# Moving the transposes of one more pair of heads from TensorE to VectorE and DMAs, and scoring one group a product earlier

## The reference

```
scores = cap * tanh(q @ k.T / sqrt(64) / cap)
attn   = exp(scores - max) / (sum + 1e-9);  x = attn @ v    # heads joined: (4*448, 768)
h = sigmoid(x @ w_gate) * (x @ w_val)                       # d_ff 1536   first product
z = h @ moe_w_out                                           # 768         second product
g = z @ moe2_w_in;  g = g * cos(g)                          # d_ff 2048   third product
y = g @ moe2_w_out                                          # 768         fourth product
```

## Time and profile before

| what | value |
|---|---|
| median of 3 runs | 1210.89 us (1210.07 to 1212.64) |
| the profiled execution, its own time | 1212.21 us |
| its span, first to last instruction | 1210.2 us |
| TensorE busy | 1199.9 us, 99% of the span |
| VectorE, ScalarE, GpSimd busy | 621.4, 508.4, 516.7 us |
| mean granted TensorE clock | 0.997 of full speed |
| moved by DMAs | 298.77 MB, mean 247 GB/s |

### The profile page before, as it was taken

The page is one execution under the profiler, slowest core; times in us unless marked ns, Lnnn a source line. Parts: engine busy times, 40 slices in busy tenths (PEclk is TensorE's granted clock), DMA queues, the critical chain, the costliest instruction groups (busy, mean ns, idle before and its releaser), DMA issues.

```text
span 1210.2 us, 16764 instructions
## 1 busy us (share of the span) xinstructions
PE 1199.9 (99%) x5932; PEld 1089.3 (90%) x5932; DVE 621.4 (51%) x1227; ACT 508.4 (42%) x957; POOL 516.7 (43%) x458
## 2 busy tenths in 40 slices
PE   8999999999999999999999999999999999999998
PEld 6779989999999999989999999999999999999998
DVE  8951148876773466766651265777662211105610
ACT  8941145656541445546640245545661011105610
POOL 7969968879753346662104406674302100000000
PEclk8999999999999999999999999999999999999999
DMA  5579987799776699999678769999768566666663
GB/s 162 161 243 317 316 308 235 241 319 321 291 284 238 224 262 259 255 262 285 235 238 272 254 194 271 263 275 258 262 227 283 191 221 216 212 221 220 239 233 108
DMA packets 150034, 298.77 MB, mean 247 GB/s; under 512 B 60480, under 2 KB 69440, under 8 KB 149952
## 3 DMA queue, kind: packets, MB, share of 16 engines
q1 hardware_dynamic: 134064, 287.37, 71.9%
q10 hardware_dynamic: 15888, 10.33, 3.2%
HBM read 219.39 MB, written 58.98 MB: 230 GB/s over the span
## 4 chain that ended last, share of the span: by engine, by line
PE 94%; ACT 2%; DVE 1%; DMA 1%; SPq 1%; issue 0%; ACTq 0%
PE acc L842 27%; PE acc L841 27%; PE acc L843 27%; PE s_ps L739 3%; PE s_ps L740 3%; PE acc L794 2%; PE t_ps L811 2%; PE t_ps L813 1%; PE t_ps L776 1%; PE acc L831 1%; PE t_ps L760 1%; PE acc L833 1%; SPq L484 1%; ACT h_lo_whole L1041 0%; DMA pt_lo_whole<-h_lo_whole 0%
## 5 line engine op out<-in xcount | busy, mean ns | idle before, releaser
L841 PE MATMUL acc<-h_hi,w_hi 128*128 128x448 f32 x672 | 247.4, 368 | 0.0
L842 PE MATMUL acc<-h_lo,w_hi 128*128 128x448 f32 x672 | 245.6, 366 | 0.0
L843 PE MATMUL acc<-h_hi,w_lo 128*128 128x448 f32 x672 | 245.5, 365 | 0.0
L841 PE MATMUL acc<-x_hi,w_hi 128*128 128x448 f32 x576 | 211.3, 367 | 0.0
L842 PE MATMUL acc<-x_lo,w_hi 128*128 128x448 f32 x576 | 211.0, 366 | 0.0
L843 PE MATMUL acc<-x_hi,w_lo 128*128 128x448 f32 x576 | 210.9, 366 | 0.0
L562 POOL TENSOR_TENSOR pt_lo<-pt_lo_whole,pt_hi 128x1344 fp32r<-128x1344 f32 x24 | 74.5, 3105 | 220.7 <-ACT pt_hi L1069 220.7
L843 PE MATMUL acc<-z_hi,w_lo 128*128 128x448 f32 x384 | 140.2, 365 | 0.0
L841 PE MATMUL acc<-z_hi,w_hi 128*128 128x448 f32 x384 | 140.2, 365 | 0.0
L842 PE MATMUL acc<-z_lo,w_hi 128*128 128x448 f32 x384 | 140.2, 365 | 0.0
L843 PEld LDWEIGHTS acc<-h_hi,w_lo 128*128 128x128 f32 x672 | 126.2, 188 | 10.1
(11 more groups left out here) (138 smaller groups left out, 1976.4 us busy)
## 6 DMA issues: line engine op xcount, KB each, us to landing
w_lo<-w_pair SPq DMA_DIRECT2D x156, 384.0 KB, 4.0
w_hi<-w_pair SPq DMA_DIRECT2D x156, 384.0 KB, 3.4
w_lo_whole<-w SPq DMA_DIRECT2D x52, 384.0 KB, 3.8
w_pair<-w_lo SPq DMA_DIRECT2D x52, 384.0 KB, 4.4
w_pair<-w_hi SPq DMA_DIRECT2D x52, 384.0 KB, 4.9
w_lo<-w_pair SPq DMA_DIRECT2D x36, 512.0 KB, 4.4
w_hi<-w_pair SPq DMA_DIRECT2D x36, 512.0 KB, 3.7
qk_in_whole<-qk SPq DMA_DIRECT2D x35, 512.0 KB, 5.9
```

Source lines behind the costliest of these rows:

```text
L841: e.matmul(out[:, 0:S], w_hi[u % HI][:, wb, :], a_hi[:, kb, :], start=first, stop=False)
L842: e.matmul(out[:, 0:S], w_hi[u % HI][:, wb, :], a_lo[:, kb, :], start=False, stop=False)
L843: return e.matmul(out[:, 0:S], w_lo[u % LO][:, wb, :], a_hi[:, kb, :], start=False, stop=last)
```

## The change

`MOVED` becomes 11: pair 11 is transposed by VectorE and moved by DMAs as well. Its blocks go to SP at the last three halves of batch 0 (`moves_of_first`), the last quarter of each head to ScalarE at steps 18 and 20. Its low parts are written by VectorE, by a `moved_low` there, not by POOL. Group 41 is scored within the third product, after its first half unit; so all later groups are scored, exponentiated and normalised one step earlier, and `prob` has two more tiles to hold them.

```diff
-MOVED = 2 * PAIRS
+MOVED = 2 * PAIRS - 1
+BETWEEN = NG * PAIRS + FOURTH_0 + AHEAD
-    prob = sb("prob", [P, TILES - 1, S])
+    prob = sb("prob", [P, TILES + 1, S])
     def scored_at(b, n):
+        if b == 0 and n >= FOURTH_0:
+            return group_of(b, n + AHEAD + 1) if FOURTH_0 < n < STEPS - AHEAD - 1 else None
+        return group_of(b, n + ahead(b)) if n + ahead(b) < STEPS else None
     def scored_before(b, n):
+        n += AHEAD if b == 0 and n >= FOURTH_0 else ahead(b) - 1
+        return group_of(b, n) if 0 <= n < STEPS else None
     def prob_of(g):
-        if g < NG * MOVED:
+        if g < NG * MOVED and g != BETWEEN + 1:
             return last_prob if ts[0] == TILES - 1 else prob[:, ts[0]:ts[-1] + 1, :]
-        at = moved_no(g) % 3 * 2
+        at = moved_no(g) % NG * 2 if g >= NG * MOVED else TILES - 1
...
 # SP, and the like in ScalarE's move_blocks
-                    e.wait_ge(s_pv, max(2 * (pr - 1) + d + 1, 2 * MOVED))
+                    e.wait_ge(s_pv, 2 * (pr - 1) + d + 1)
+                    if pr == MOVED:
+                        e.wait_ge(s_tr, TILES * MOVED)
+            def moves_of_first(n):
+                d, last = divmod(n - len(halves) + 3, 2)
+                if d >= 0:
+                    move_blocks(MOVED, d, (0, 1, 2) if d == 1 else (2,) if last else (0, 1))
...
                         if n >= KEEP_LATER:
                             keep(*halves[n - KEEP_LATER])
+                        moves_of_first(n)
...
 # TensorE
             def times_v(b, i, d):
-                    g = NG * i + 3 + d 
+                    g = NG * i + 3 + d + (NG * i >= FOURTH_0)
             def third_product(b):
                         m.then_inc(s_acc, 1)
+                        if b == 0 and j == 0 and h == 0:
+                            e.wait_ge(s_tanh, BETWEEN + 1)
+                            scores(BETWEEN + 1, s_ps)
...
 # ScalarE, attend
-                if b > 0 and n % 2 == 0 and 0 <= n + 2 < STEPS and n != FOURTH:
+                if n % 2 == 0 and 0 <= n + 2 < STEPS and pair_of(b, (n + 2) // NG) >= MOVED and (b == 0 or n != FOURTH):
                     move_last_blocks(b, n)
 # ScalarE, end of second_product
-                    tanh(group_of(b, FOURTH_0 + AHEAD))
+                    tanh(BETWEEN)
+                    tanh(BETWEEN + 1)
...
 # VectorE
+            def moved_low(pr, d):
+                e.wait_ge(s_pbhi, 2 * (pr - MOVED) + d + 1)
+                at = of_head(d)
+                e.tensor_tensor(pt_lo[:, 0:CH, at], pt_whole[:, 0:CH, at], f32(pt_hi)[:, 0:CH, at],
+                                ALU.subtract).then_inc(s_pblow, 1)
+                e.wait_ge(s_pblow, 2 * (pr - MOVED) + d + 1)
+                e.tensor_tensor(pt_hi[0:D, CH, at], pt_whole[D:P, CH, at], f32(pt_hi)[D:P, CH, at],
+                                ALU.subtract).then_inc(s_pb, 1)
             def attend(b, n):
+                i, r = divmod(n, NG)
+                if b == 0 and NG * MOVED <= group_of(b, n + AHEAD - 1) < group_of(b, STEPS):
+                    turn_blocks(group_of(b, n + AHEAD - 1))
+                if b == 0 and i < PAIRS and pair_of(b, i) >= MOVED and r in (1, 3):
+                    moved_low(pair_of(b, i), r // 2)
...
 # VectorE, end of second_product
-                    row_max(group_of(b, last + 1))
+                    row_max(BETWEEN)
+                    row_max(BETWEEN + 1)
```

More of the change, by code:

```diff
@@ L288, in scored_at @@
     def scored_at(b, n):
-        return group_of(b, n + ahead(b)) if n + ahead(b) < STEPS and (b > 0 or n != FOURTH_0) else None
+        if b == 0 and n >= FOURTH_0:
+            return group_of(b, n + AHEAD + 1) if FOURTH_0 < n < STEPS - AHEAD - 1 else None
+        return group_of(b, n + ahead(b)) if n + ahead(b) < STEPS else None
     def scored_before(b, n):
-        return group_of(b, n + ahead(b) - 1) if 0 <= n + ahead(b) - 1 < STEPS and (b > 0 or n != FOURTH_0) else None
+        n += AHEAD if b == 0 and n >= FOURTH_0 else ahead(b) - 1
+        return group_of(b, n) if 0 <= n < STEPS else None
     def step_of(b, stage, j, h):
@@ L328, in prob_of, with last_there @@
         ts = GROUPS[g % NG]
-        if g < NG * MOVED:
+        if g < NG * MOVED and g != BETWEEN + 1:
             return last_prob if ts[0] == TILES - 1 else prob[:, ts[0]:ts[-1] + 1, :]
-        at = moved_no(g) % 3 * 2
+        at = moved_no(g) % NG * 2 if g >= NG * MOVED else TILES - 1
         return prob[:, at:at + len(ts), :]
+    def last_there(g):
+        return {BETWEEN + 1: g - 2 * NG, BETWEEN + 1 + NG: g - 2 * NG, BETWEEN + 3 + NG: BETWEEN + 1}.get(g, g - NG)
     def turned_by_tensor(b, n):
@@ L920, in third_product @@
                             e.wait_ge(s_o, 2 * (pair_of(b, PAIRS // 2 - 1) - ALONE) + h + 1)
-                            e.wait_ge(*normalised(tiles_of(group_of(b, FOURTH_0 + AHEAD - 1))[-1]))
+                            e.wait_ge(*normalised(tiles_of(BETWEEN - 1)[-1]))
                         else:
@@ L986, in _ @@
                 if b == 0:
-                    between = group_of(b, FOURTH_0 + AHEAD)
-                    e.wait_ge(s_tanh, between)
-                    scores(between, s_ps)
+                    e.wait_ge(s_tanh, BETWEEN)
+                    scores(BETWEEN, s_ps)
                 third_product(b)
@@ L1014, in tanh @@
                 e.wait_ge(s_score, g + 1)
-                if moved_no(g) >= 3:
-                    e.wait_ge(s_blocks, moved_no(g) - 3 + 1)
+                if moved_no(g) >= NG:
+                    e.wait_ge(s_blocks, moved_no(g) - NG + 1)
                 elif g >= NG * (ALONE + 1):
-                    e.wait_ge(s_tr, tiles_of(g - NG)[-1] + 1)
+                    e.wait_ge(s_tr, tiles_of(last_there(g))[-1] + 1)
                 e.activation(prob_of(g), at[:, 0:len(ts), 0:S], ACT.Tanh,
@@ L1108, in attend @@
                         x_high(pr)
-                i, r = divmod(n + 1, NG)
-                if b > 0 and 0 <= i < PAIRS and r in (0, 2) and i != FOURTH // NG:
+                i, r = divmod(n + 1 if b > 0 else n, NG)
+                if 0 <= i < PAIRS and r in (0, 2) and pair_of(b, i) >= MOVED and i != first_of_fourth(b) // NG:
                     moved_high(pair_of(b, i), r // 2)
@@ L1150, in second_product @@
                 if b == 0:
-                    exp(group_of(b, FOURTH_0 + AHEAD - 1))
+                    exp(BETWEEN - 1)
                 z_high(b, U2 - 1)
@@ L1409, in second_product @@
                 if b == 0:
-                    last = FOURTH_0 + AHEAD - 1
-                    normalise(group_of(b, last), zeros[0])
-                    row_max(group_of(b, last + 1))
+                    normalise(BETWEEN - 1, zeros[0])
+                    row_max(BETWEEN)
+                    row_max(BETWEEN + 1)
             def third_product(b):
```

## The result

The changed kernel takes 1222.3 us (median of 6 runs, 1219.8 to 1225.4), the kernel before 1211.7 in the same comparison: a ratio of 1.0091 (95% interval 1.0071 to 1.0111), 10.6 us slower. The direction was forecast; the size was not: +3.2 was predicted, and 1222.3 lies above the range of 1209.2 to 1218.2. The profiled execution took 1222.1 us with a span of 1220.3, against 1210.2 before.

What follows compares the result with a forecast made beforehand. TensorE, busy 1199.9 of 1210.2 us, bounds the kernel. Late weights for batch 1's second half unit give +3.2, holding the 2.7 saved and step 13's wait: 1215.4 against the profiled run, 1214.1 against the median; range 1209.2 to 1218.2.

Steps and rivals of the forecast that it cites:

- What can be gained, 2.7 us: TensorE's stream loses 25 transposes of pair 11 at 0.11 us each: 2.7 us, 0.23% of the time.
- The rival of 6.8 us: Each of the 25 transposes costs its full 273 ns on TensorE, 6.8 us saved, total 1207.3; chance 0.02.
- Step 12, a wait of 1.9 us more: ScalarE's exponential ahead of the high parts makes TensorE's transposes at step 13 wait 1.9 us more (1.1 to 2.3).
- The blocks ready at 354.3, SP's queue waiting for them: SP's first moves of pair 11 wait for VectorE's turn of group 45 until 354.3, with loads and keeps behind.
- SP's chain: SP issues moves, loads and keeps from 354.3; last keeps start at 372.6, all kept at 382.6, 11.5 us later.
- My upper bound: SP and weights: 0.7 us an issue, VectorE 1.7 later, keeps 11 us, what follows 11.5: a loss of 8 us.
- Step 21, a wait of 0.3 us (0 to 3): TensorE waits 0.3 us for head 0's low part, ready at 371.5, hidden in the later wait for weights.
- The waits for weights, 0.7 and some 3 us: TensorE waits for DMAs at batch 1's first and second half units, 0.7 and some 3 us.
- a sign of being wrong: The prediction counts as wrong if TensorE waits at steps 21 and 23; size not given.
- the small pieces fill the DMA queues: Pair 11's moves in 448-byte pieces run at half rate, delaying blocks and keeps: +5 to +8, say 1217.5; chance 0.08.
- It cancels: SP, the keeps or VectorE are quicker, weights come between 388.5 and 392.6: within 2.4 us of before, say 1211; chance 0.32.
- the moves are hidden: All keeps pass before 377.5, no weights late, step 12 costs under 0.3 us: 2.4 to 2.7 gained, 1208.3; chance 0.11.

Runs made afterwards that it cites:

- Kernel ten: Kernel of eight, but batch 1's loads wait only for their own unit's and buffer's keeps, and group 40's normalisation reads other zeros: 1209.8 us, ratio 0.9985.
- experiment nine: Kernel of eight, but all three last keeps are issued behind head 1's moves, where two stood ahead: 1215.7 us, ratio 1.0032.
- experiment two: Changed kernel, but TensorE takes head 0's product with v one step later, at step 22: 1223.1 us, ratio 1.0091.
- seven: Changed kernel with last loads and two keeps no longer behind all pair 11 moves, and step 12's high parts before the exponential: 1216.3 us, ratio 1.0039.
- eight: Kernel of seven, but head 0's product with v comes a step later, at step 22: 1211.8 us, ratio 0.9998.
- experiment one: Changed kernel, but batch 1's loads wait only for their own unit's and buffer's keeps, last three keeps spread over three half units: 1219.4 us, ratio 1.0065.
- third kernel: Changed kernel with the edits of experiment one and experiment two together: 1218.3 us, ratio 1.0053.
- five: Changed kernel with SP's order altered: the last two loads and their keeps no longer stand behind all pair 11 moves: 1218.0 us, ratio 1.0051.
- the fourth: Only the earlier scoring of group 41 and later groups; TensorE transposes pair 11 as before: 1214.2 us, ratio 1.0023 against the kernel before.

## Why the prediction was right in its direction and wrong in its size

- *What can be gained, 2.7 us:* right as far as it can be seen. Kernel ten has the transposes gone and nearly no new wait, and its -1.8 (-0.4 to -3.3) agrees with 2.4. The rival of 6.8 us is outside.
- *Step 12, a wait of 1.9 us more:* right: 2.0 us of waits against 0.2, and for the reason given. The exponential now stands ahead of the high parts:

```profile
314.18 0.77 ACT L1045 ACTIVATE prob<-prob,shift,cap_abs 128x448 f32<-128x448 f32 x1
...
315.68 0.48 ACT L1083 ACTIVATE pt_hi<-t_ps 128x384 fp32r<-128x384 f32 x1
```

  The fall of the clock that can follow such a wait was not in the sum.
- *The blocks ready at 354.3, SP's queue waiting for them:* right, 355.1. The window of 350 to 355 us shows the cost of the idle queue, a DMA share of 0.00 in the changed kernel:

```profile
350.00:355.00 5.00, 5.00 (x28) 4.61 (x27) 4.87 (x12) 2.02 (x5) 2.97 (x2) 1.00 0.00 0
```

- *SP's chain, the term that failed:* I let 24 moves take 15.5 us at the 0.64 to 0.7 us of the earlier trace rows wherever they stood. They took 5.3 + 4.3 + 9.8 = 19.3, since sixteen of them followed weight DMAs that still filled the queues, as experiment nine shows. With small terms besides (0.8 at the start, 1.1 in the loads, keeps and gaps) the last keeps came at 378.3, not 372.6, and with 0.5 more in the drain the loads at 388.7, not 382.6: 6.1 us late of what was forecast. That is most of the 7.4 us by which the total was too low. The largest part is 3.8 us of issues, and the earlier trace rows already held the sign of it: behind 1.5 MB issued from 339.46 on, the load at 340.94 took 1.24 us to issue, where the one at 339.46 took 0.43. My upper bound took 0.7 us an issue, so it did not hold the size either. The half unit's weights after that took 10.3 us (10.8 forecast), and the next half units kept up, as forecast. Some 1.3 us more are lost later, which the sum did not have.
- *Step 21, a wait of 0.3 us (0 to 3):* wrong, 5.1, and 2.0 for the clock. My sum let head 0's high part start when its blocks had landed, 367.5; it started at 371.0, since it had no term for ScalarE's four moves for head 1, 4.7 us, which stand ahead of it. And it had the low part at 1.6 us, which is right for VectorE alone (1.54) but not beside POOL (3.36). In the total it is hidden by the weights, as I wrote of a wait below 1 us, and as experiment two shows of one of 5. It comes due as soon as the weights are on time (seven against eight).
- *The waits for weights, 0.7 and some 3 us:* 0 and 1.8. The weights were later than forecast, but TensorE, held at step 21, was later too. A wait at step 21 was named as a sign of being wrong, and it came.
- *Rivals:* "the small pieces fill the DMA queues" had the right place and came nearest in size, +5 to +8 against +10.6, for the wrong reason: the large weight DMAs ahead slow the issues, not the moves' own pieces; with nearly empty queues the same 448-byte pieces are issued at 0.64 us and the DMA share is 0.25. Per byte the pieces do take more of the DMA engines, 54 GB/s at a share of 0.25 against 300 at 0.82, but at that share there is room. "It cancels" and "the moves are hidden" needed a quicker chain on SP; it was slower.

Open: the cause of the waits beside later batches in kernel seven's profile, and of the last 1.3 us in the changed kernel's. Part of the changed kernel's spread of 6 us is probably the clock: its two runs of 1225.4 us had a mean granted clock of 0.992 and 0.993, the other four, 1219.8 to 1222.5, had 0.996. By estimate from these, 0.0035 less over 1222 us is about 4 us, if TensorE was busy while the clock was low.

## What to carry to other kernels

Before a wait goes into a queue that issues DMAs, list what stands behind it: here two loads and three keeps had 20 and 11 us of slack each, and bunching them cost more than what the change saved. Price an issue by what fills the DMA queues when it is made, and price it again on every engine that issues. Where two late chains meet at nearly the same time, mend both before judging either: the step that gave 0 us alone was worth 4.5 once the other was gone.

## What the runs showed of the hardware

- An issue of a 42 or 56 KB DMA takes 0.64 us on SP with nearly empty queues and up to 1.07 just behind 1.5 MB of weights (changed kernel); on ScalarE 0.71 and up to 1.24 (4.94 us for four, kernel ten). An instruction behind such issues waits with them.
- VectorE's subtraction of two SBUF operands (128x1344) takes 1.54 us alone and took 3.36 beside POOL's subtraction and copy; POOL's 0.41 us copy took 1.71 then. Beside POOL's cast it took 1.56, and the cast 2.09 instead of 1.05 (experiment one).
- A wait of TensorE of 5.1 us was followed by 4 us at half the granted clock (2.0 us lost). In the third kernel two waits of 1.2 and 0.7 us, with three transposes between them, were followed by such a stretch too (1.6 us lost); the same two waits in the changed kernel and in kernels one, two and five (1.2 to 1.3 and 0.7 us), and those of 1.0 and 0.7 us in the fourth, were not.
